# Two slots of a pair of weight slices in place of four slots of one

## What is computed

```
attn = softmax(q k^T / 8 + bias(i, j)) v            8 heads of 64, sequence 576
x    = attn, as 2304 x 512
h    = max(x @ w1, x @ w2, x @ w3)                   512 -> 768
x    = h @ w_out                                     768 -> 512
h    = x @ w_in                                      512 -> 2048      "second layer"
g    = where(h >= 1, h, where(h <= -1, 0, (h + 1)^2 / 4))
out  = g @ w_out2                                    2048 -> 512
```

## Time and profile before

| | |
|---|---|
| three runs | 1012.41, 1012.89, 1014.35 us; median 1012.89 |
| profiled execution | 1012.26 us, its span 1010.2 us |
| busy | PE 98%, PEld 89%, DVE 61%, ACT 50%, POOL 36% of the span |
| TensorE clock granted, mean | 0.996 of full |
| moved by DMA | 169.71 MB, 168 GB/s over the span |
| stage D | from about 613.6 us to the end |

### The profile page before, as it was taken

One profiled execution on the slowest core, in us unless ns is written; L12 is line 12 of the kernel. 1 busy time (PEld: TensorE's weight loads), 2 busy tenths in 40 slices (PEclk: granted clock), 3 DMA queues, 4 the chain that ended last, 5 costly groups with the idle time before them and its releaser, 6 DMA issues.

```text
span 1010.2 us, 23289 instructions
## 1 busy us (share of the span) xinstructions
PE 987.5 (98%) x8832; PEld 895.8 (89%) x8832; DVE 611.6 (61%) x1509; ACT 508.4 (50%) x1032; POOL 366.3 (36%) x634
## 2 busy tenths in 40 slices
PE   6979999999999999999999999999999999999998
PEld 4557777777777999999999999999999999999998
DVE  8957667667683232314231315777777877778776
ACT  8968788787793321212121213555545444545543
POOL 1049888888874796887720000000000000000000
PEclk9989999999999999999999999999999999999999
DMA  5882534425311456446550056976666666666772
GB/s 126 256 257 59 154 73 106 125 49 157 98 34 58 139 168 235 170 178 215 210 228 0 0 220 234 354 251 191 223 198 208 218 200 214 195 216 188 224 219 73
DMA packets 122725, 169.71 MB, mean 168 GB/s; under 512 B 67072, under 2 KB 84736, under 8 KB 120960
## 3 DMA queue, kind: packets, MB, share of 16 engines
q1 hardware_dynamic: 122528, 168.37, 53.2%
q10 hardware_dynamic: 96, 0.00, 0.0%
HBM read 129.64 MB, written 38.70 MB: 167 GB/s over the span
## 4 chain that ended last, share of the span: by engine, by line
PE 79%; DVE 1%; DMA 0%; ACT 0%; issue 0%; DVEq 0%
PE ps L1285 22%; PE ps L1350 20%; PE ps L1376 17%; PE ps L1312 7%; PE ps L1236 5%; PE ps L1176 4%; PE ps L1197 2%; PE ps L1211 1%; PE ps L1150 1%; DMA w_all<-win_scratch 0%; DVE s_sb L936 0%; DVE tb L1112 0%; DVE g_lo L1127 0%; ACT tb L874 0%; ACT g_hi L888 0%
## 5 line engine op out<-in xcount | busy, mean ns | idle before, releaser
L1285 PE MATMUL ps<-x_hi,w_all 128*128 128x384 f32 x864 | 225.9, 335 | 1.2 <-ACT ta L820 1.2
L1350 PE MATMUL ps<-x_hi,w_all 128*128 128x256 f32 x1152 | 219.2, 283 | 0.8 <-DMA w_all<-win_scratch 0.8
L1350 PEld LDWEIGHTS ps<-x_hi,w_all 128*128 128x128 f32 x1152 | 184.8, 192 | 1.0 <-DMA w_all<-win_scratch 1.0
L1376 PE MATMUL ps<-w_all,g_hi 128*128 128x256 f32 x1008 | 184.6, 283 | 0.2 <-DVE g_lo L1127 0.2
L1350 PE MATMUL ps<-x_lo,w_all 128*128 128x256 f32 x576 | 163.0, 283 | 0.0
L1285 PEld LDWEIGHTS ps<-x_hi,w_all 128*128 128x128 f32 x864 | 156.7, 188 | 2.9 <-DVE xT L957 1.7
L1376 PEld LDWEIGHTS ps<-w_all,g_hi 128*128 128x128 f32 x1008 | 157.2, 192 | 0.4 <-DVE g_lo L1127 0.4
L936 DVE CUSTOM_DVE_ANT_0 s_sb<-ps,bias_h 128x576 f32<-128x576 f32 (+1 forms) x160 | 114.8, 753 | 69.9 <-PE ps L1176 52.1
L1285 PE MATMUL ps<-x_lo,w_all 128*128 128x384 f32 x432 | 144.3, 334 | 0.0
L1376 PE MATMUL ps<-w_all,g_lo 128*128 128x256 f32 x504 | 142.6, 283 | 0.0
L592 POOL TENSOR_SCALAR probs<-probs,row_inv 128x576 f32<-128x576 f32 (+1 forms) x160 | 120.2, 761 | 19.3 <-DVE row_inv L966 18.7
(11 more groups left out here) (119 smaller groups left out, 1821.4 us busy)
## 6 DMA issues: line engine op xcount, KB each, us to landing
w_all<-win_scratch SPq DMA_DIRECT2D x144, 512.0 KB, 4.4
wt_scratch<-w_all SPq DMA_DIRECT2D x8, 1792.0 KB, 6.8
bias_scratch<-p_t SPq DMA_DIRECT2D x36, 296.0 KB, 4.5
w_all<-wt_scratch SPq DMA_DIRECT2D x5, 1792.0 KB, 7.5
win_scratch<-w_all SPq DMA_DIRECT2D x8, 1024.0 KB, 6.5
raw<-in_moe_w_out SPq DMA_DIRECT2D x22, 256.0 KB, 7.1
w_all<-wt_scratch SPq DMA_DIRECT2D x12, 448.0 KB, 6.8
bias_h<-bias_scratch SPq DMA_DIRECT2D x16, 288.0 KB, 4.5
```

The source lines that it names most:

```text
L1285: last = pe.matmul(ps[:, bank, 0:BLK], w[:, at:at + P], x[:, kt, :], start=(kt == 0 and n == 0), stop=(kt == KT - 1 and n == 2))
L1350: last = pe.matmul(ps[:, n_bank(n), f * SBT:(f + 1) * SBT], w_all[:, at + lo:at + lo + P], x[:, s, :], start=(kt == 0 and i == 0), stop=(k ...
L1376: last = pe.matmul(ps[:, bank, 0:HD], x[:, n % 2, g * P:(g + 1) * P], w_all[:, at + lo:at + lo + HD], start=(j == 0 and m == 0), stop=(j = ...
```

## The change

A slot now holds a pair of slices, and there are two slots. One transfer of 1024 KB fetches both slices of item n. It waits until both slices of item n - 2 are used up, and PE waits once for each item, ahead of its first slice. The two semaphores `win_in` alternate by item. Where slices were followed by quarters of the output weights, a pair is now followed by two quarters; the stores of a block come behind the pair that holds slices 10 and 11.

```
-        win_in = [sem(f"win_in{r}") for r in range(WRING)]
+        win_in = [sem(f"win_in{r}") for r in range(WRING // 2)]
...
-            def load_win(k):
-
-                if k >= WRING:
-                    sp.wait_ge(d_in, k - WRING + 1)
-                sp.dma_start(w_all[:, ring_at(k):ring_at(k) + WIN].bitcast(F32),
-                             win_d[k % NF2]).then_inc(win_in[k % WRING], 16)
+            def load_win(n):
+
+                at, j = ring_at(2 * n), n % NPAIR
+                if n >= WRING // 2:
+                    sp.wait_ge(d_in, 2 * n - WRING + 2)
+                sp.dma_start(w_all[:, at:at + 2 * WIN].bitcast(F32).rearrange("p (f c) -> p f c", f=2),
+                             win_d[2 * j:2 * j + 2].rearrange("f p c -> p f c")).then_inc(win_in[n % 2], 16)
...
-            for m in range(WRING):
+            for m in range(WRING // 2):
                 load_win(m)
...
-            for m in range(WRING, NF2 * NSB):
-                load_win(m)
-                for j in PIECES:
-                    if m in PIECES[j]:
-                        load_wt(j, PIECES[j][m], 4)
-                if m >= NF2 and m % NF2 == 10:
-                    store_out(m // NF2 - 1)
+            for n in range(WRING // 2, ND):
+                load_win(n)
+                for m in (2 * n, 2 * n + 1):
+                    for j in PIECES:
+                        if m in PIECES[j]:
+                            load_wt(j, PIECES[j][m], 4)
+                if n >= NPAIR and n % NPAIR == 5:
+                    store_out(n // NPAIR - 1)
...
-                    pe.wait_ge(win_in[k % WRING], 16 * (k // WRING + 1))
+                    if f == 0:
+                        pe.wait_ge(win_in[n % 2], 16 * (n // 2 + 1))
```

## The result

| | before | changed |
|---|---|---|
| median, twelve runs each | 1012.12 us (1011.49 to 1014.35) | 1014.14 us (1012.87 to 1017.10) |
| ratio | | 1.0024, 95% interval 1.0013 to 1.0035 |
| profiled execution, its span | 1012.26, 1010.2 us | 1013.99, 1012.1 us |
| granted TensorE clock, mean | 0.996 | 0.993 |

The changed kernel is slower by 0.24%. The time lies within the predicted range, but it is just over the 0.2% up to which I had called it no change. The interval stands for 1.3 to 3.5 us, so these runs alone can't tell the 1.5 us that I forecast from the larger losses of the rivals. The traces can.

The account below looks back on a forecast made before the run. PE was taken to bound the kernel, in a dense row absorbing no delay. Item 2's later start, 1.5 us, was the only nonzero term: 1012.89 + 1.5 = 1014.4 us, counted as no change; range 1013.2 to 1016.3.

Parts of the forecast that it names:

- the larger losses of the rivals: Slower cases: clock falling in item 2's wait, 1016.1 us, chance 0.08; pair slower than two halves, 1015.8 us, chance 0.15.
- The place: Item 2, the first transfer after the first layer: the only term that counts, +1.5 us; waits and issues elsewhere cost 0.
- the dense stretch: Items 4 to 9, where the DMA queue is always busy: price 0, with the thinnest slack at item 9.
- The predicted slack at item 9: Pair 9 lands at 658.7 and is needed at 660.26, everything shifted by 1.5: slack 1.6 us.
- The size of the wait: At item 2, PE starts 1.5 us later; the stall grows from 0.83 to about 2.3 us.
- The 6.15 us for 1 MB: Skill page's time for a 1 MB transfer; by that estimate the kernel would take 1015.5 us.
- the bound from the stores: Upper bound at item 2: 1024 KB stores take 5.1 to 6.8 us, giving a start up to 3.2 us later.
- The clock: Rival: clock drops to half level for about 3.4 us at item 2's wait, costing 1.7 us more, 1016.1; chance 0.08.
- the likeliest case: Forecast of 1.5 us at item 2 with the clock staying at 1.00: 1013.9 to 1015.0 us, chance 0.62.
- signs of being wrong: Several pair waits between 630 and 665, first pair landing over 5.6 or below 4.6 us, or matmul steps other than 0.12.
- A pair slower than two halves: Rival: a 1024 KB transfer lands like the stores, in 6.5 us; item 2 costs 2.9 us, 1015.8; chance 0.15.
- costs less than its second half: Rival: item 2's pair lands 0.5 us sooner, costing 1.0 us, in the extreme 1012.1 us; chance 0.12.

Follow-up runs that it names:

- experiment 1: Changed kernel with only item 2's pair fetched as two 512 KB transfers, a wait ahead of each slice: 1011.99 us, ratio 0.9997 to the kernel before.
- Experiment 2: Changed kernel with 16 matmuls on operands at hand put ahead of item 2's products, filling the wait: 1013.20 us, ratio 1.0009 to the kernel before.
- experiment 6: Changed kernel with 8 matmuls filling part of the wait at item 2: 1013.83 us, ratio 1.0011 to the kernel before.
- 10: Changed kernel with 3 matmuls in the wait at item 2: 1014.86 us, ratio 1.0020 to the kernel before.
- experiment 3: Kernel before, 512 KB transfers and four slots kept, but PE waits for slices 4 and 5 together ahead of item 2: 1015.12 us, ratio 1.0034.
- 4: Changed kernel with item 2's pair issued ahead of SP's wait for the first layer's last output products: 1012.26 us, ratio 0.9998 to the kernel before.
- experiment 9: The changed kernel profiled and timed once more, nothing altered: 1014.66 us, ratio 1.0018 to the kernel before.

## Why the prediction was right or wrong

**What bounds the kernel** was right: the loss is what PE was made to wait and what followed, and the dense row took back nothing.

**The place** was right. One wait for a transfer, at item 2, and no other. Items 3 to 71, the dense stretch and the stores cost nothing. The predicted slack at item 9 was 1.6 us, and it was 1.4; that nothing was left of it in experiment 1 shows that calling it the thinnest was right.

**The size of the wait** was close. The sum had PE start 1.5 us later. The last product of item 1 starts at 621.26 before and at 620.39 in the changed kernel, so a dense row would go on 0.12 us later, at 621.38 and 620.51. From there to the start of item 2 it is 622.37 - 621.38 = 0.99 before and 622.83 - 620.51 = 2.32 us changed, that is 1.33 more. The pair landed in 4.9 us, not in 5.1 to 5.2. Experiment 2 puts this term at 1.20 us and experiment 6 at 1.32. The estimate from the page of the Trainium skill "DMA: Bandwidth & Descriptors", section "Anatomy of one DMA", was 1.2; both are near enough that neither decides. The 6.15 us for 1 MB of its section "Bandwidth" are not borne out here, and both sections give their figures for transfers issued from GpSimd, while SP issues these. Nor is the bound from the stores borne out: reads of that size took 4.7 to 7.1 us in the changed kernel, and the one at item 2, with nothing ahead of it, 4.9.

**The clock** is where the likeliest case failed. I named this rival, with place and mechanism, and gave it 0.08. It happened in both profiles of the changed kernel. The step that failed is the argument against it: "PE is fully busy on both sides of this wait, and the present 0.83 us leave the clock at 1.00". The first half is true and protects nothing: PE is as fully busy on both sides in all these kernels, and only the idle stretch between differs in experiments 2, 6 and 10. The second half is an inference from 0.83 us to 2.3 us, while the row at hand with a wait of that size, 2.23 us, had the clock fall behind it. I set that row aside because PE was less busy ahead of it. The nearest row in the length of the wait was the better guide. One of my own signs of being wrong, matmuls that step by more than 0.12 us, came true at item 2. The rival's price, 1.7 us, was also slightly off. Its measured size is 1.49 us from the products of item 2 and 1.52 us between experiments 6 and 10. The 3.4 us at the lower level were right. But at half clock a matmul of 256 columns steps by 0.64 / 3 = 0.213 us, and not by twice 0.12, so the time at the lower level isn't lost by a full half.

The Trainium skill's page "TensorE: Matmul & The Clock Gate", section "Part 1: The HAM clock gate", says that an idle stretch sends the clock to its lower level. That holds here with 1.76 us and more of idle time, and doesn't with 1.2 us and less.

**The sum.** With its own rows the wait and the clock give 1.33 + 1.49 = 2.82 us, against 2.79 us in the tails and 2.0 us between the medians. The rival as priced gave 1016.1 from a base of 1012.9. On the base of the twelve runs, 1012.1, it is 1015.3 against 1014.1 measured. The forecast came within 0.3 us of the measured median by luck: it left out a term of 1.49 us, the kernel before measured 0.8 us lower in the longer series, and the medians differ by 0.8 us less than the tails. Two small sums of the prediction are off as well. By its own words (1.0 us less half a microsecond, on 1012.89) the range begins at 1013.4 and not at 1013.2, and the 6.15 us of the page lead to 1015.4 and not to 1015.5. Neither matters for the result.

**The other rivals.** A pair slower than two halves fell in experiment 3: the same loss without pairs. That it costs less than its second half (1.0 us) isn't borne out either, though by little: the 1.33 us lie nearer to 1.5.

## What to carry to other kernels

When a transfer is made larger and the consumer waits for all of it, the place to look is not the steady state but the first use behind a point where the queue was held back: there the whole second half is on the path. If the wait grows towards two microseconds, price the matmuls behind it at the lower clock too, and take the nearest row by the length of the wait. And before a fetch is made earlier, look for who else is nearly as late: here the gain came only once ACT's chain was let go as well.

## What the hardware showed that I had not expected

**Idle time costs more than itself.** A wait of 1.2 us costs 1.2 us. One of 1.76 us is followed by a fall of the clock that costs 1.5 us more (experiments 6 and 10). So the first 8 filling matmuls of experiment 6, 1.0 us of useless work, save 1.5 us.

**Instruction fetch in the last stores.** In experiments 1, 4 and 9 the time from the last matmul to the end of the span is 5.3, 5.0 and 5.3 us, where all other profiles have 4.3 to 4.4. SP's timeline of experiment 9, which is the changed kernel once more, shows one issue of 1.45 us among the last stores:

```profile
1008.95 1.45 SPq L519 DMA_DIRECT2D out<-raw  x1
```

Its table of DMA queues for that stretch (packets, MB, share) has one instruction fetch:

```profile
q8 instruction: 1, 0.02, 3.3%
```

In the first profile of the same kernel the issue takes 0.43 us, and its fetch of that size lies some 3 us earlier, between 1006.0 and 1006.5:

```profile
1009.32 0.43 SPq L519 DMA_DIRECT2D out<-raw  x1
```

In experiments 1, 4 and 9 the fetch lies 0.2 to 0.3 us ahead of the long issue (1.47, 1.23 and 1.45 us). In all the other profiles none lies in the 2.5 us ahead of that issue, and it takes 0.43 to 0.44 us. The same program thus pays it in one execution and not in another. It falls behind all the work of the kernel, so it made the span 0.7 to 1.0 us longer each time. That the fetch delays the issue is read from their lying together; no run took it away.
